# Block transposes of a mixture-of-experts stage written into PSUM, a second buffer for the split input rows, and the token tables put behind the first steps

## The reference, cut to what matters

```python
def _moe_ref(x, w_gate, w_output_gate, w1, w2) -> np.ndarray:
    logits = x @ w_gate
    e_idx = np.argmax(logits, axis=1)
    logits_s = logits - logits.max(-1, keepdims=True)
    probs = np.exp(logits_s)
    probs /= probs.sum(-1, keepdims=True) + 1e-09
    gate_w = probs[np.arange(N), e_idx]
    eom = 1.0 / (1.0 + np.exp(-(x @ w_output_gate)))
    for e in range(E):
        mask = e_idx == e
        h = np.maximum(x[mask] @ w1[e], 0.0)
        ye = h @ w2[e]
        out[mask] = gate_w[mask, None] * eom[mask, e, None] * ye
```

## Time and profile before

| what | us |
|---|---|
| median of 3 runs | 1077.05 |
| lowest and highest run | 1075.08 and 1082.54 |
| the profiled execution | 1083.84 |
| its span | 1082.1 |
| PE busy in the span | 1037.4 |
| DVE busy | 722.2 |
| ACT busy | 312.7 |
| POOL busy | 390.9 |

### The profile page before, as it was taken

The page is one execution under the profiler, slowest core; times in us unless marked ns, Lnnn a source line. Parts: engine busy times, 40 slices in busy tenths (PEclk is TensorE's granted clock), DMA queues, the critical chain, the costliest instruction groups (busy, mean ns, idle before and its releaser), DMA issues.

```text
span 1082.1 us, 18080 instructions
## 1 busy us (share of the span) xinstructions
PE 1037.4 (96%) x5424; PEld 864.3 (80%) x5425; DVE 722.2 (67%) x1247; ACT 312.7 (29%) x560; POOL 390.9 (36%) x325
## 2 busy tenths in 40 slices
PE   9999968989999999999789999999999999999998
PEld 8888857878888888787678887888887888888887
DVE  3666674654655556555478768877787886887775
ACT  2222212322323222231123333333334333333333
POOL 4377768585585995935700000000000000000000
PEclk9999988999999999999989999999999999999999
DMA  9898747776777886864200010001001001000101
GB/s 332 278 315 307 254 152 223 223 240 213 242 234 223 273 262 221 259 204 165 81 10 11 20 39 19 19 0 48 19 10 48 16 13 39 19 0 0 40 1 39
DMA packets 70964, 138.28 MB, mean 128 GB/s; under 512 B 7056, under 2 KB 39184, under 8 KB 70928
## 3 DMA queue, kind: packets, MB, share of 16 engines
q1 hardware_dynamic: 21888, 73.41, 20.5%
q10 hardware_dynamic: 45200, 51.82, 14.9%
q0 software_dynamic: 3840, 12.59, 3.6%
HBM read 98.73 MB, written 39.06 MB: 127 GB/s over the span
## 4 chain that ended last, share of the span: by engine, by line
PE 80%; DVE 8%; DMA 6%; issue 2%; ACTq 1%; ACT 1%; POOL 0%; DVEq 0%; SPq 0%; POOLq 0%
PE banks L1114 15%; PE banks L1116 15%; PE banks L1115 15%; PE banks L1206 8%; PE banks L1208 8%; PE banks L1207 8%; DMA hid_rows<-hid 2%; PE banks L1009 2%; PE banks L1053 2%; PE banks L1042 2%; DMA xs_sb<-x_sorted 2%; PE banks L1019 2%; PE banks L1027 2%; DVE xsT_lo L825 1%; DVE hidT L866 1%
## 5 line engine op out<-in xcount | busy, mean ns | idle before, releaser
L382 POOL TENSOR_TENSOR w_sb<-raw,w_sb 128x1024 fp32r<-128x1024 f32 x80 | 197.4, 2468 | 6.7
L395 POOL DMA_INDIRECT gathered<-y_sorted,row_back x20 | 22.5, 1127 | 375.7 <-DVE x_sb L926 375.0
L1206 PE MATMUL banks<-x2T_hi,w_sb 128*128 (+1 forms) x384 | 153.0, 398 | 5.1 <-DVE g_sb L961 5.1
L1208 PE MATMUL banks<-x2T_lo,w_sb 128*128 (+1 forms) x384 | 150.7, 392 | 0.0
L1207 PE MATMUL banks<-x2T_hi,w_sb 128*128 (+1 forms) x384 | 150.5, 392 | 0.0
L1116 PE MATMUL banks<-w_sb,g_hi 128*128 128x512 f32 x384 | 149.4, 389 | 0.0
L1114 PE MATMUL banks<-w_sb,g_lo 128*128 128x512 f32 x384 | 149.4, 389 | 0.0
L1115 PE MATMUL banks<-w_sb,g_hi 128*128 128x512 f32 x384 | 149.4, 389 | 0.0
L1114 PE MATMUL banks<-w_sb,xsT_lo 128*128 (+1 forms) x248 | 100.8, 406 | 19.2 <-DVE xsT_lo L825 19.0
L633 ACT ACTIVATE square<-banks 128x512 f32<-128x512 f32 x96 | 57.4, 597 | 195.7 <-PE banks L1208 195.7
L640 ACT ACTIVATE g_hi<-g_sb 128x512 fp32r<-128x512 f32 x96 | 60.7, 632 | 164.5 <-PE banks L1116 146.8
(11 more groups left out here) (129 smaller groups left out, 1834.1 us busy)
## 6 DMA issues: line engine op xcount, KB each, us to landing
raw<-in_weights SPq DMA_DIRECT2D x80, 512.0 KB, 4.1
in_sb<-in_rows SPq DMA_DIRECT2D x48, 512.0 KB, 6.5
hid_rows<-hid ACTq DMA_DIRECT2D x31, 512.0 KB, 3.3
hid_quads<-hid_rows ACTq DMA_DIRECT2D x31, 512.0 KB, 4.3
xs_sb<-x_sorted ACTq DMA_DIRECT2D x124, 64.0 KB, 3.1
y_sorted<-ys_sb ACTq DMA_DIRECT2D x31, 256.0 KB, 3.1
out_rows<-out_sb SPq DMA_DIRECT2D x24, 256.0 KB, 2.2
x_sorted<-zeros ACTq DMA_DIRECT2D x1, 2048.0 KB, 20.5
```

The lines of the kernel that those rows point to most:

```text
L382: nc.gpsimd.tensor_tensor(w_sb[:, s, 1, lo:hi], raw[:, p % RAW_SLOTS], w_sb[:, s, 0, lo:hi].bitcast(fp32), ALU.subtract).then_inc(piece_do ...
L1206: T.matmul(out_, w_lo, hi, start=first, stop=False)
L1208: return T.matmul(out_, w_hi, lo, start=False, stop=last)
```

## The change

- `xsT` and `hidT` leave SBUF. Both become banks of PSUM: bank 0 for `xsT`, banks 3 and 6 for the halves of `hidT`. DVE's transposes write there, and the instructions that make the high and low parts read from there. PE's dummy matmuls that wrote bank 0 write bank 1.
- `xsT_hi` and `xsT_lo` get two buffers, taken in turn by tiles. x_hi(i+1) now waits for the end of hidden(i-1) instead of standing behind the second relu of step i.
- The lists change. In step i, ACT: **x_hi(i+1)**, relu(i, first half), store_rows(i-3), relu(i, second half), store_hidden(i), hid_hi(i-1), load_hidden(i), load_rows(i+2). DVE: **transpose_rows(i+1), x_lo(i+1)**, copy_rows(i-3), transpose_hidden(i-1), hid_lo(i-1).
- DVE's chain of small instructions is cut in four groups that stand behind steps 0, 1, 2 and 3; ACT's two Exp stand behind its step 0.

The first `moe_step` in the diff is ACT's, the second DVE's.

```diff
-    xsT = c_.place("xsT", [P, DK, P])
-    xsT_hi = c_.place("xsT_hi", [P, DK, P], fp32r)
-    xsT_lo = c_.place("xsT_lo", [P, DK, P], fp32r)
+    xsT_hi = c_.place("xsT_hi", [P, 2, DK, P], fp32r)
+    xsT_lo = c_.place("xsT_lo", [P, 2, DK, P], fp32r)
...
-    hidT = c_.place("hidT", [P, FK, P])
...
+        xsT = at(0)
+        hidT = [at(3), at(6)]
...
-            def x_hi(i):
+            def x_hi(i, number):

                 act.wait_ge(xsT_done, i + 1)
-                nc.scalar.activation(xsT_hi[:].rearrange("p a n -> p (a n)"), xsT[:].rearrange("p a n -> p (a n)"), ACT.Copy)\
+                if number >= 2:
+
+                    act.wait_ge(hid_done, i * 2 - 2)
+                nc.scalar.activation(xsT_hi[:, number % 2].rearrange("p a n -> p (a n)"), xsT, ACT.Copy)\
...
             def moe_step(i, number):

+                if number + 1 < MOE_TILES:
+                    x_hi(i + 1, number + 1)
                 relu(i, 0)
                 if number >= 3:
                     store_rows(i - 3)
                 relu(i, 1)
                 store_hidden(i, number)
-                if number + 1 < MOE_TILES:
-                    x_hi(i + 1)
                 if number >= 1:
                     hid_hi(i - 1, number - 1)
                 load_hidden(i)
                 if number + 2 < MOE_TILES:
                     load_rows(i + 2)
...
+            moe_step(0, 0)
             act.wait_ge(shifted_done, 1)
             nc.scalar.activation(shifted[:], shifted[:], ACT.Exp).then_inc(exp_done, 1)
             nc.scalar.activation(per_tile[1][:], per_tile[0][:], ACT.Exp, scale=-1.0).then_inc(exp_done, 1)
-            for i in range(3):
+            for i in range(1, 3):
                 moe_step(i, i)
...
             def moe_step(i, number):
+                if number + 1 < MOE_TILES:
+                    transpose_rows(i + 1)
+                    x_lo(i + 1, (number + 1) % 2)
                 if number >= 3:
                     if number >= 4:

                         dve.wait_ge(ys_stored, i * 16 - 48)
                     copy_rows(i - 3)
-                if number + 1 < MOE_TILES:
-                    transpose_rows(i + 1)
                 if number >= 1:
                     transpose_hidden(i - 1)
-                if number + 1 < MOE_TILES:
-                    x_lo(i + 1)
-                if number >= 1:
                     hid_lo(i - 1, (number - 1) % 2)
-            for i in range(5):
-                moe_step(i, i)
+            moe_step(0, 0)
+            gate_scores()
+            moe_step(1, 1)
+            token_scales()
+            moe_step(2, 2)
+            rows_before()
+            moe_step(3, 3)
+            rows_after()
+            moe_step(4, 4)
```

More of the change, by code:

```diff
@@ L574, in hid_hi @@
                     nc.scalar.activation(hidT_hi[:, number % 2, cols].rearrange("p a n -> p (a n)"),
-                                         hidT[:, cols].rearrange("p a n -> p (a n)"), ACT.Copy).then_inc(hidT_hi_done, 1)
+                                         hidT[n], ACT.Copy).then_inc(hidT_hi_done, 1)
             def relu(i, n):
@@ L600, in _ @@
             load_rows(0, first=True)
-            x_hi(0)
+            x_hi(0, 0)
             act.wait_ge(tables_done, 1)
             load_rows(1)
+            moe_step(0, 0)
             act.wait_ge(shifted_done, 1)
@@ L819, in transpose_rows, with x_lo @@
                     dve.wait_ge(xsT_lo_done, i)
-                V.transpose(xsT[:].rearrange("p k (g b) -> p g k b", g=QUADS),
+                V.transpose(xsT.rearrange("p (k g b) -> p g k b", k=DK, g=QUADS),
                             xs_sb[:].rearrange("p g (k a) -> p g k a", k=DK)).then_inc(xsT_done, 1)
-            def x_lo(i):
+            def x_lo(i, par):
                 dve.wait_ge(xsT_hi_done, i + 1)
-                V.tensor_tensor(xsT_lo[:].rearrange("p a n -> p (a n)"), xsT[:].rearrange("p a n -> p (a n)"),
-                                xsT_hi[:].rearrange("p a n -> p (a n)").bitcast(fp32), ALU.subtract).then_inc(xsT_lo_done, 1)
+                V.tensor_tensor(xsT_lo[:, par].rearrange("p a n -> p (a n)"), xsT,
+                                xsT_hi[:, par].rearrange("p a n -> p (a n)").bitcast(fp32), ALU.subtract).then_inc(xsT_lo_done, 1)
@@ L829, in _ @@
             transpose_rows(0, first=True)
[L830 to L847, removed]
@@ L848, in _ @@
-            over_tokens = [P, TOKEN_TILES, EXPERTS]
[L849 to L857, removed]
+            x_lo(0, 0)
+            over_tokens = [P, TOKEN_TILES, EXPERTS]
+            def gate_scores():
+                link(V.tensor_tensor(gate_all[:], output_gate, onehot[:], ALU.mult))
+                link(V.reduce_sum(per_tile[0][:], gate_all[:], AX))
+                V.tensor_tensor(shifted[:], router, over_experts(top[:]), ALU.subtract).then_inc(shifted_done, 1)
@@ new lines, in token_scales @@
+            def token_scales():
+                dve.wait_ge(exp_done, 2)
+                link(V.reduce_sum(top[:], shifted[:], AX))
+                link(V.tensor_scalar(top[:], top[:], 1e-9, None, ALU.add))
+                link(V.tensor_scalar(per_tile[1][:], per_tile[1][:], 1.0, None, ALU.add))
+                link(V.reciprocal(top[:], top[:]))
+                link(V.reciprocal(per_tile[1][:], per_tile[1][:]))
+                link(V.tensor_tensor(token_scale[:], top[:], per_tile[1][:], ALU.mult))
@@ new lines, in rows_before @@
+            def rows_before():
+                first_tile, move = per_expert[0], per_expert[7]
+                link(V.tensor_tensor(first_tile[:], through[:], tiles[:], ALU.subtract))
+                link(V.scalar_tensor_tensor(out=move[:], in0=first_tile[:], scalar=float(P), in1=region_row,
+                                            op0=ALU.mult, op1=ALU.subtract))
+                link(V.tensor_tensor(gate_all[:], move[:].unsqueeze(1).to_broadcast(over_tokens), onehot[:], ALU.mult))
+                link(V.reduce_sum(per_tile[0][:], gate_all[:], AX))
+                link(V.tensor_tensor(per_tile[0][:], per_tile[0][:], row_at[:], ALU.add))
@@ new lines, in rows_after @@
+            def rows_after():
+                link(V.tensor_tensor(gate_all[:], last_start[:].unsqueeze(1).to_broadcast(over_tokens), onehot[:], ALU.mult))
+                link(V.reduce_sum(per_tile[1][:], gate_all[:], AX))
+                link(V.tensor_scalar(tile_row[:], row_at[:], ROW_BITS - (P - 1), None, ALU.bitwise_and))
+                link(V.tensor_tensor(per_tile[1][:], tile_row[:], per_tile[1][:], ALU.subtract))
+                V.scalar_tensor_tensor(out=row_back[:], in0=per_tile[1][:], scalar=0.0, in1=per_tile[0][:],
+                                       op0=ALU.max, op1=ALU.add).then_inc(rows_back_done, 1)
@@ L865, in transpose_hidden @@
                     ks = slice(n * DK, (n + 1) * DK)
-                    V.transpose(hidT[:, ks].rearrange("p k (b g) -> p g k b", g=QUADS),
+                    V.transpose(hidT[n].rearrange("p (k b g) -> p g k b", k=DK, g=QUADS),
                                 hid_quads[:].rearrange("p g (k a) -> p g k a", k=FK)[:, :, ks]).then_inc(hidT_done, 1)
@@ L1106, in _ @@
             rank(TOKEN_TILES - 2)
-            stay_warm(WARM_TAIL[1], still, 0)
+            stay_warm(WARM_TAIL[1], still, 1)
             rank(TOKEN_TILES - 1)
@@ L1116, in split_product, with hidden @@
                 return T.matmul(out_, hi, w_lo, start=False, stop=last)
-            def hidden(i, first=False):
+            def hidden(i, par, first=False):
                 if first:
@@ L1132, in hidden @@
                         lo = (n * DK + k) * WIDE
-                        last = split_product(at(1 + n), xsT_hi[:, k], xsT_lo[:, k],
+                        last = split_product(at(1 + n), xsT_hi[:, par, k], xsT_lo[:, par, k],
                                              slot_part(slot, 0, lo, lo + WIDE), slot_part(slot, 1, lo, lo + WIDE),
@@ L1152, in rows_out @@
                 last.then_inc(ys_done, 1)
-            stay_warm(WARM_TAIL[2], still, 0)
-            stay_warm(WARM_TAIL[3], still, 0)
-            hidden(0, first=True)
+            stay_warm(WARM_TAIL[2], still, 1)
+            stay_warm(WARM_TAIL[3], still, 1)
+            hidden(0, 0, first=True)
             pe.wait_ge(tables_done, 1)
-            hidden(1)
+            hidden(1, 1)
             def moe_step(i, number):
-                hidden(i)
+                hidden(i, number % 2)
                 rows_out(i - 2, number, number % 2)
@@ L1170, in _ @@
                 if i < MOE_TILES:
-                    hidden(i)
+                    hidden(i, i % 2)
                 rows_out(i - 2, i, i % 2)
```

2 lines of the change are left out of this document (1 added, 1 removed).

## The result

The changed kernel takes 1159.78 us, the median of 4 runs from 1157.49 to 1163.13. The kernel before took 1079.6 in the runs beside it. The ratio is 1.0752, with a 95% interval of 1.072 to 1.0785: 7.5% slower, 80 us. The prediction was 1146, 69 us more than before. The profiled execution of the changed kernel took 1160.97 us with a span of 1159.2, 1.2 us above its median. The profiled execution of the kernel before, 1083.84 us, lies 4.2 us above the 1079.6, so differences between profiles and differences between medians need not be the same to a few microseconds.

What follows compares the result with a forecast made beforehand. PE was taken to set the pace before; afterwards ACT's loop, 2.5 + 10.2 + 1.35 = 14.05 us a step, delays hidden(30) by 71.0 us, less 2 given back: +69, so 1146 us. Forecast 1125 to 1166, wider range 1102 to 1170.

Steps and rivals of the forecast that it cites:

- the chain from the second relu to the next x_hi: ACT's loop through hid store, loads, landing and transpose closes within one step: 14.05 us, where PE needs 10.9.
- the hold of the second relu by the y store: In ACT's list, store_rows(i-3) waits for copy_rows behind x_lo, so the second relu ends 2.5 us after x_hi, not 1.2.
- PE's wait ahead of rows_out for copy_rows: PE waits for ys_sb ahead of rows_out some 25 times, 2 to 4 us each; a sign of being right.
- d: Time from the end of step i's second relu to the landing of tile i+2's rows; forecast 10.2 us, 8.8 to 10.9.
- what is given back behind it: At the stage's end the two hidT_lo take 2.99 us where two of 0.68 would do; 2 us given back.
- two corrections: On d: the weights' share falls from 2.7 to 2.3 us in longer steps; the y store adds up to 0.4 us.
- the one on the clock: PE's half-clock falls cost 2.8 us each, covered by 3.15 us slack a step; the end moves by at most a microsecond.
- The faster one: Rival, chance 0.06: the lists cost nothing, only PE's gaps go; 1054 us; needs d under 6.2 us.
- The one of no change: Rival, chance 0.04: with d at 7.8 us in every step the loop gives back just what the start gains.
- The milder loss by a hold that does not happen: Milder-loss rival, chance 0.20 for both forms: the y store does not hold the second relu; 34 us less, 1112.
- the one by a d of 8.8: Milder-loss rival, chance 0.20 for both forms: transfers clash less in longer steps, d falls to 8.8; 40 us less, 1106.
- The larger loss by a transpose of 1.08 us or a stretched x_lo: Rival, chance 0.10: x_lo at 0.90 or above, or slow transpose, d at 10.9; 1182 with all three, 1166 to 1172 with two.

Runs made afterwards that it cites:

- e2: The changed kernel with copy_rows(i-3) put back to the head of DVE's list, nothing else; 1118.4 us, ratio to before 1.035.
- e3: The changed kernel with ACT's load_rows(i+2) moved from the end of the step to right behind x_hi(i+1); 1066.6 us, ratio to before 0.987.
- e9: The changed kernel with load_rows(i+2) moved two places forward, to right behind store_hidden(i); 1082.4 us, ratio to before 1.0017.
- e1: The changed kernel with ACT's and DVE's lists put back as before; PSUM, two buffers and four groups stay; 1066.5 us, ratio to before 0.9855.
- e4: The changed kernel with each weight load of the expert stage and after cut to 64 of 1024 columns, so results are wrong; 1099.6 us, ratio to before 1.0172.
- e5: The kernel before with only xsT and hidT moved to PSUM and the dummy matmuls to bank 1; 1070.9 us, ratio to before 0.9923.

## Why the prediction was right

**The place of the loss.** The prediction named the chain from the second relu to the next x_hi, the hold of the second relu by the y store, and PE's wait ahead of rows_out for copy_rows. All three are in the waits after the change. e2 takes away the hold alone, e3 opens the chain and e9 shortens it, and e1 undoes all of it. PE's wait for copy_rows, 51.6 us after the change, is gone from e1, e2 and e3 and 9.6 us in e9. It came 18 times at 2.9 us in the mean, where some 25 were forecast: behind short steps PE hardly waits.

**The terms.**

| term | predicted, us | measured, us |
|---|---|---|
| tile 1's first matmul | 151.2 | 151.98 |
| x_hi(2) ends | 163.3 | 163.7 |
| x_hi to the end of the second relu | 2.5 | 2.6, in the mean 2.8 |
| d | 10.2 | 10.06 |
| landing to the end of x_hi | 1.35 | 1.45 |
| x_hi(30) ends | 554.1 | 560.6 |
| hidden(30) ends | 566.5 | 574.1 |
| what is given back behind it | 2 | 0.4 |

Tile 1 started 0.8 us late because hidden(1) also needs both relus of tile 0, which I had left out:

```profile
151.98 0.49 PE L1132 MATMUL banks<-w_sb,xsT_lo 128*128 x1 [0.89 <-ACT hid L583]
```

d was sized by two corrections, less for the weights and more for the y store. e4 leaves 2.1 us for the weights, where 2.3 had been reckoned and 2.7 taken for the kernel before. The y store's share was measured by no run; that the sum came out within 0.14 us owes something to luck.

**The number.** The forecast of 1146 is 13.8 us under the median. 8.1 of these lie in the profile (1160.97 for 1152.8): x_hi(30) came 6.5 us late, hidden(30) another 1.1, and the end gave back 0.4 us for 2, while the dense stage took 1.2 us less which stays unexplained. The other 5.6 us have nothing to do with the lists: I took 6.8 us off for the distance of the profiled execution from the median, and for the changed kernel that distance is 1.2. It is a property of one execution and does not carry over.

**The step that fell short** is the one on the clock. I held that PE's falls to half clock stay covered, at no more than a microsecond in all. In the 28 steps the clock fell to its lower level 13 times, not at every turn. The stretch was granted 0.92 and PE was busy for 337.2 us in it with the same 1344 matmuls that took 311.4 before. Nearly all of that was covered indeed, as long as d was long. But a fall and a short d follow each other. After PE's 10 us of idle time that ended at 194.6, ACT's timeline of the changed kernel reads:

```profile
204.55 0.60 ACT L554 ACTIVATE xsT_hi<-banks 128x512 fp32r<-128x512 f32 x1 [7.12 <-DVE banks L824]
205.35 0.60 ACT L583 ACTIVATE hid<-banks 128x512 f32<-128x512 f32 x1 [0.20 <-PE banks L1134]
...
208.07 0.60 ACT L583 ACTIVATE hid<-banks 128x512 f32<-128x512 f32 x1 [2.12 <-PE banks L1134]
```

Here the second relu waits for PE and ends 3.5 us behind x_hi instead of 2.6, since hidden(4) came late out of the slow stretch. In six of the 26 long steps it is so, by 0.5 to 1.3 us, 4.8 us in sum. They are just the six steps in which d was under 8.2 us and the clock was granted at its lower level for a part; the six others with so short a d, at full clock, have 2.6, and so have the long ones with a fall. With no fall PE's way from copy_rows through rows_out and hidden to the second relu (1.5 + 10.9 + 0.65 = 13.05 us) would be 1.4 us shorter than ACT's even in a short turn (2.6 + 7.8 + 1.45 + 2.6 = 14.45); a fall takes more than that. In e4, where d is short throughout and the clock stands at 0.99, the second relu ends 2.6 to 2.8 us behind x_hi in every long step. A loop worked out with a mean d hides this: its long turns are long, and its short ones are cut off by the other engine. To these 4.8 us come the start (0.4), the transpose into PSUM and the starts (0.1 us a step, 2.8 in all) and the relu's 0.1 us (2.3); the d that was 0.14 us shorter than forecast took 3.9 back. That makes the 6.5 us that x_hi(30) came late, to 0.1. Of the 86 us by which the 28 steps grew, the clock explains no more than the 4.8. Behind it hidden(30) came another 1.1 us later than reckoned.

**What was given back at the end** was over-sized. The two `hidT_lo` did shrink from 2.99 us to 1.3, but PE's wait ahead of the last rows_out fell only from 1.43 us to 1.02. What it waits for is copy_rows, which can't begin before PE has done the rows_out in front:

```profile
509.25 0.49 PE L1114 MATMUL banks<-w_sb,hidT_lo 128*128 x1 [1.43 <-DVE ys_sb L881]
```

```profile
586.59 0.69 DVE L894 COPY ys_sb<-banks 128x512 f32<-128x512 f32 x1 [2.28 <-PE banks L1134]
```

```profile
587.51 0.49 PE L1132 MATMUL banks<-w_sb,hidT_lo 128*128 x1 [1.02 <-issue]
```

The first line is of the kernel before. There the second `hidT_lo` held the copy on DVE for the 0.4 us; the rest of its 2.99 us ran beside PE's matmuls.

**The rivals.** The faster one asked for d under 6.2 us; the shortest d was 7.6. The one of no change got its own run, e4, and came out at 1.7% over. The milder loss by a hold that does not happen is e2's size, 41 us against 34; the one by a d of 8.8 did not come, as d fell by 0.4 us only. The larger loss by a transpose of 1.08 us or a stretched x_lo did not come: 0.73 and 0.69. Its sum was wrong in one place: two of its three parts give 1162 to 1176 us, not 1166 to 1172.

## What to carry to other kernels

When work is moved to the head of an in-order list, look at what issues its input: if the load is issued at the end of the same list, the list has become a loop with the transfer inside it, and its length has to be worked out against the pace of the bound engine. A second buffer buys nothing as long as the load that feeds it is issued at the end of the step before; here moving that load by two places was worth 77 us, moving it to the head or undoing the lists 93, and no run shows a gain from the buffer itself. Split a change into its parts before judging it: the PSUM part was worth 9 us and was carried under by the order of two lists.

## What the runs showed of the hardware

- A DVE block transpose that writes every fourth element took 1.08 us for 128x512 into SBUF and 0.70 into PSUM. In e5, where only the place was changed, it took 0.68. The one that writes 32 neighbours took 0.71 and 0.73. So for these two shapes the strided target costs 0.37 us in SBUF and nothing in PSUM.
- The DVE subtraction `xsT_lo` with one operand in PSUM took 0.666 to 0.693 us in e1 and the changed kernel, with POOL at work beside it or not. With both in SBUF it took up to 2.6 us: the 16 of the 31 that took 0.90 us or more all ran beside POOL's L382, and the 9 with no instruction of POOL beside them took 0.655 to 0.693. No run changed POOL's work.
- The 64 KB loads landed in 2.4 us (median) with the weight loads cut, and in 3.1 with them.
